# Waits of TensorE placed so that nearly every matmul has one, in a fused attention and two-layer feed-forward kernel

## Chip, cores and metric

The kernel runs on one core of a Trainium2 chip. The metric is the device time of one execution in microseconds (us), lower is better. TensorE does the matmuls and has its weight loads shown as an engine of their own (PE and PEld in the profile); VectorE is DVE, ScalarE is ACT, GpSimd is POOL, SyncE is SP.

## The reference

```python
# q, k, v: (4, 8, 576, 64)
scores = where(block_i >= block_j, 0.125 * q @ k.T, -1e9)      # blocks of 64 rows and columns
attn = exp(scores - max(scores)); attn /= sum(attn) + 1e-9
x = (attn @ v).transpose(0, 2, 1, 3).reshape(2304, 512)
h = x @ moe_w_in                                               # (512, 2048)
x = where(h >= 1, h, where(h <= -1, 0, (h + 1) ** 2 / 4)) @ moe_w_out
h = x @ moe2_w_in
out = (h * cos(h)) @ moe2_w_out
```

## The kernel before

Each operand of a matmul is split in a high and a low fp32r part, and every product is made from two or three matmuls of such parts (high by high, high by low, low by high). ACT makes the high parts, DVE or POOL the low ones.

**Attention.** A head's 576 rows are taken in two items: rows 0 to 255 (an early item, n = 0 to 31, score tiles 0 and 1) and rows 256 to 575 (a late item, n = 32 to 63, score tiles 2, 3 and 4). An item goes through `score` (queries by keys, in PSUM), row maximum (DVE), exponential with row sum (ACT, L616), reciprocal (DVE), scaling (POOL, L513), `turn` (TensorE transposes, L1019), the split of the transposed probabilities (ACT `pt_hi`, DVE `pt_lo`, L817), `weigh` (probabilities by values, L1036), and the addition of the two halves into the feed-forward's input (DVE, which then counts up `heads_read`). A late item has three transpose groups, `turn(n, 0)`, `turn(n, 1)` and `turn(n, 2)`; the third writes the PSUM tile `turned` that the first wrote. The low part of the queries is made by DVE (`q_lo_made`, L789), that of the keys by POOL (`k_lo_made`, L506).

**Feed-forward.** Tokens go in tiles of 256, t = 0 to 8 in the first layer, t = 9 to 17 in the second. The hidden dimension is taken in eight pairs of 128-blocks; a tile is 32 units on TensorE, four for a pair: two that make a hidden pair (`make_hidden`, L1090, 12 matmuls in each), and two that use one (`use_hidden`; first layer L1115, 12 matmuls in each; second layer L1107, six of 512 columns in each). Making runs two pairs ahead of using (LAG). The second layer's tiles 9 to 16 are one hardware loop.

**Order.** Every engine executes its instructions in the order in which its code is written. The steps of an item have slots in a table (AT), one table for all engines; the first nine items run alone, the others beside the tiles 0 to 6: `slots_beside` spreads the slots over half units, and TensorE calls `beside_half` in the middle (before matmul 6) and at the end of a unit. For a late item, `score` of tiles 2 and 3 is at slot 0, tile 4 at slot 7, `turn(n, 2)` at slot 19, which is slot 0 of the next item and comes before that item's scores.

## Time and profile before

| what | value |
|---|---|
| median of 3 runs | 1044.55 us (1042.11 to 1044.83) |
| the profiled execution | 1051.79 us |
| its span, first to last instruction | 1049.6 us |
| mean granted TensorE clock | 0.981 of full speed |
| instructions | 19879 |
| PE busy | 1001.9 us (95%), 7360 matmuls |
| PEld busy | 943.1 us (90%), 7360 weight loads |
| DVE, ACT, POOL busy | 657.0, 590.8, 426.5 us |

The three timed runs are taken without the profiler, the profiled execution is a further one. A matmul's row begins when its operand is read and ends by a model; rows of neighbouring matmuls overlap, so the distance between their starts is the time that one takes of the engine. A semaphore instruction's row is listed by its line and is not counted as busy.

### The profile page before, as it was taken

What the parts mean: (1) busy time and instruction counts of PE and PEld (TensorE: products, weight loads), DVE (VectorE), ACT (ScalarE), POOL (GpSimd) and SP (SyncE); (2) the same over time, 40 slices, a digit from 0 to 9 for tenths busy, and PEclk for the clock granted to TensorE, in tenths of its full rate; (3) what the DMA queues carried; (4) which work ended last, traced back from release to release, by engine and by line L of the source; (5) the groups of instructions that cost most, each with busy time, mean ns of one, the idle gap of its engine ahead of it and who ended that gap; (6) DMA issues with size and microseconds to landing.
All of it is one profiled execution on the core that took longest, in us unless ns stands there. A gap on an engine that the chain in (4) does not pass through costs nothing.

```text
span 1049.6 us, 19879 instructions
## 1 busy us (share of the span) xinstructions
PE 1001.9 (95%) x7360; PEld 943.1 (90%) x7360; DVE 657.0 (63%) x1422; ACT 590.8 (56%) x1232; POOL 426.5 (41%) x446
## 2 busy tenths in 40 slices
PE   4688999999999999999999999999999999999997
PEld 3578999999999999999999998999999999999995
DVE  5567777766766767666732378656565555656553
ACT  5567776766666666666633356544444444445442
POOL 3559765555555554655522221222222222222211
PEclk9579999999999999999999999999999999999999
DMA  4335321221211212121200144010110101001000
GB/s 133 104 118 157 98 90 65 72 70 49 92 49 53 89 49 72 70 72 65 69 31 22 41 161 162 1 40 0 40 40 0 40 0 40 21 19 40 0 21 21
DMA packets 30886, 62.28 MB, mean 59 GB/s; under 512 B 3680, under 2 KB 11872, under 8 KB 30816
## 3 DMA queue, kind: packets, MB, share of 16 engines
q1 hardware_dynamic: 29664, 57.16, 17.1%
q10 hardware_dynamic: 1152, 4.19, 1.1%
q8 instruction: 43, 0.70, 0.3%
q14 instruction: 27, 0.22, 0.1%
HBM read 51.90 MB, written 9.44 MB: 58 GB/s over the span
## 4 chain that ended last, share of the span: by engine, by line
PE 79%; DVE 9%; ACT 5%; issue 3%; POOL 1%; DMA 1%; ACTq 0%; POOLq 0%; DVEq 0%
PE hidden L1090 33%; PE acc L1107 18%; PE acc L1115 12%; PE heads_out L1036 4%; PE scores L1001 4%; PE turned L1019 3%; PE scores L1002 3%; DVE neg_max L800 1%; PE heads_out L1019 1%; DVE x_lo L879 1%; PE hidden L1073 1%; DVE wout_lo L865 1%; DVE work L885 1%; ACT probs L616 1%; DVE pt_lo L817 1%
## 5 line engine op out<-in xcount | busy, mean ns | idle before, releaser
L543 POOL TENSOR_TENSOR g_lo<-work,g_hi 128x512 fp32r<-128x512 f32 x144 | 187.9, 1305 | 450.7 <-ACT g_hi L713 450.7
L1090 PE MATMUL hidden<-x_hi,win_hi 128*128 128x256 f32 x1136 | 323.5, 285 | 2.8 <-DVE work L912 1.2
L1090 PE MATMUL hidden<-x_hi,win_lo 128*128 128x256 f32 x1136 | 317.9, 280 | 0.0
L1090 PE MATMUL hidden<-x_lo,win_hi 128*128 128x256 f32 x1136 | 317.9, 280 | 0.0
L1090 PEld LDWEIGHTS hidden<-x_hi,win_hi 128*128 128x128 f32 x1136 | 214.3, 189 | 7.6 <-issue 2.0
L1090 PEld LDWEIGHTS hidden<-x_lo,win_hi 128*128 128x128 f32 x1136 | 214.2, 189 | 3.3
L1090 PEld LDWEIGHTS hidden<-x_hi,win_lo 128*128 128x128 f32 x1136 | 216.4, 190 | 0.0
L1115 PE MATMUL acc<-g_hi,wout_hi 128*128 128x256 f32 x576 | 167.4, 291 | 0.3 <-ACT y_stage L696 0.3
L1115 PE MATMUL acc<-g_lo,wout_hi 128*128 128x256 f32 x576 | 160.6, 279 | 0.0
L1115 PE MATMUL acc<-g_hi,wout_lo 128*128 128x256 f32 x576 | 160.5, 279 | 0.0
L513 POOL TENSOR_SCALAR probs<-probs,row_inv 64x576 f32<-64x576 f32 (+2 forms) x160 | 107.4, 675 | 121.6 <-DVE row_inv L812 120.8
L723 ACT ACTIVATE work<-work 128x512 f32<-128x512 f32 x72 | 45.5, 632 | 140.3 <-DVE work L902 140.3
L616 ACT ACTIVATE probs<-scores,neg_max 64x576 f32<-64x576 f32 (+2 forms) x160 | 90.5, 567 | 58.6 <-DVE neg_max L800 56.5
L1107 PE MATMUL acc<-wout_hi,g_hi 128*128 128x512 f32 x288 | 113.7, 395 | 1.6 <-POOL g_lo L543 1.6
L1107 PE MATMUL acc<-wout_hi,g_lo 128*128 128x512 f32 x288 | 113.4, 394 | 0.0
L1107 PE MATMUL acc<-wout_lo,g_hi 128*128 128x512 f32 x288 | 112.6, 391 | 0.0
L1115 PEld LDWEIGHTS acc<-g_hi,wout_hi 128*128 128x128 f32 x576 | 108.9, 189 | 1.2 <-issue 0.4
L1115 PEld LDWEIGHTS acc<-g_lo,wout_hi 128*128 128x128 f32 x576 | 109.2, 190 | 0.6
L912 DVE TENSOR_TENSOR work<-hidden,work 128x512 f32<-128x512 f32 x72 | 49.8, 692 | 94.9 <-ACT work L725 94.9
L1115 PEld LDWEIGHTS acc<-g_hi,wout_lo 128*128 128x128 f32 x576 | 108.9, 189 | 0.0
L713 ACT ACTIVATE g_hi<-work 128x512 fp32r<-128x512 f32 x144 | 89.8, 624 | 14.7 <-DVE work L890 12.3
L800 DVE TENSOR_REDUCE neg_max<-scores 64x1 f32<-64x576 f32 (+2 forms) x160 | 86.8, 543 | 17.7 <-PE scores L1002 13.1
(91 smaller groups left out, 1830.1 us busy)
## 6 DMA issues: line engine op xcount, KB each, us to landing
qk_raw<-qk_late SPq DMA_DIRECT2D x32, 448.0 KB, 3.2
qk_raw<-qk_early SPq DMA_DIRECT2D x32, 256.0 KB, 2.6
v_raw<-v_late SPq DMA_DIRECT2D x32, 160.0 KB, 3.3
x_raw<-x_scratch SPq DMA_DIRECT2D x9, 512.0 KB, 3.5
out<-y_stage SPq DMA_DIRECT2D x36, 128.0 KB, 2.4
x_raw<-w_in SPq DMA_DIRECT2D x8, 512.0 KB, 3.6
y_stage<-w_out SPq DMA_DIRECT2D x8, 512.0 KB, 3.5
x_scratch<-y_stage ACTq DMA_DIRECT2D x8, 512.0 KB, 2.7
```

The costliest lines, as they stand in the source:

```text
L513: nc.gpsimd.tensor_scalar(tile, tile, row_inv[0:rows_of(i), col:col + 1], 1.0, ALU.mult, ALU.mult).then_inc(probs_made, 1)
L543: nc.gpsimd.tensor_tensor(g_lo[:, m % G_RING, :], work[:, m % 2, :], g_hi[:, m % G_RING, :], ALU.subtract).then_inc(g_lo_made, 1)
L616: nc.scalar.activation(tile, scores_tile(n, i), ACT.Exp, bias=neg_max[0:rows_of(i), col:col + 1], accum_out=row_sum[0:rows_of(i), col:col ...
L713: nc.scalar.activation(g_hi[:, m % G_RING, :], work[:, m % 2, :], ACT.Copy).then_inc(g_hi_made, 1)
L723: nc.scalar.activation(work[:, m % 2, :], work[:, m % 2, :], ACT.Abs).then_inc(angle_abs, 1)
L800: nc.vector.tensor_reduce(out=neg_max[0:rows_of(i), col:col + 1], in_=scores_tile(n, i), axis=AX_XY if i == 4 else AX_X, op=ALU.max, negat ...
L912: nc.vector.tensor_tensor(work[:, m % 2, :], hidden[:, m % 2, :], work[:, m % 2, :], ALU.mult).then_inc(hidden_read, 1)
L1001: nc.tensor.matmul(into, q_tile, k_hi_of(n)[:, first:end], start=True, stop=False)
L1019: last = nc.tensor.transpose(turned_of(n, e)[:, at:at + q], probs_chunk(n, i, j), ident[0:q, 0:q])
L1090: last = nc.tensor.matmul(into, w[:, p, c, half * P:(half + 1) * P], x[:, c, :], start=(i == 0), stop=(i == len(products) - 1))
L1107: last = nc.tensor.matmul(acc[:, a, :], g[:, slot, at:at + P], w[:, p, half, :], start=(p == 0 and half == 0 and i == 0), stop=(end and i ...
L1115: last = nc.tensor.matmul(into, w[:, p, half, d * P:(d + 1) * P], g[:, slot, half * TOK:(half + 1) * TOK], start=(p == 0 and half == 0 and ...
```

## The change

The waits of TensorE are placed anew; the matmuls, their order, and all other engines' code stay as they are.

- `score`: the keys' wait comes first and only ahead of an item's first tile; the queries' wait goes one matmul ahead for items from 9 on, and is left out for late items after the first, where the `pt_lo` wait of the item before (ahead of its `turn(n, 2)`) comes later in DVE's order than the queries' low part. The exponential's wait for the banks is left out where DVE's order implies it; the third tile keeps its own.
- `turn`: it waits for the scaled probabilities alone. Its second wait is left out for the first group, and goes one matmul ahead for the second (`heads_read`) and the third (`pt_lo`).
- `weigh`: the wait for `heads_read` is left out; that for the values goes one matmul ahead for items 9 to 31 and is left out for late ones.
- `make_hidden`: the wait for the activation of the pair two before (`hidden_read`) goes two matmuls ahead of the first, into the unit before. `use_hidden` of pair 0: the wait for `g_lo` goes two matmuls ahead, and the one for the accumulator (`acc_read`) stays.
- Second layer's weights: the waits at the start of the loop's body become one ahead of the loop and two single ones within it.

`steps_ahead` holds the attention's waits; it is called ahead of the matmul before a half unit's attention steps.

```diff
--- before.py
+++ after.py
@@ -111,6 +111,20 @@
 def user_before(n):
     return n - 2 if n < ALONE else n - 1
+def banks_seen(n):
+    before = n - 2 if n < ALONE else n - 1
+    last = "inv_c" if late(before) else "inv_b"
+    return n < 2 or slot_of(last, before) - sum(slots_of(m) for m in range(before, n)) <= slot_of("q_lo", n)
+def queries_seen(n):
+    return n > HEADS and slot_of("q_lo", n) + slots_of(n - 1) < slot_of("pt_lo", n - 1) and (
+        slot_of("turn_c", n - 1) <= slots_of(n - 1))
 def near(n, k):
@@ -982,15 +996,17 @@
         def _(pe):
             def score(n, i):
                 e = i - tiles_of(n)[0]
-                pe.wait_ge(q_lo_made, n + 1)
-                pe.wait_ge(k_lo_made, n + 1)
-                if late(n):
-                    pe.wait_ge(exp_made, first_tile(n) + (2 if i == 4 else 0))
-                elif n > ALONE:
-                    pe.wait_ge(exp_made, first_tile(n - 1) + e + 1)
-                elif n > 1:
-                    pe.wait_ge(exp_made, first_tile(n - 1 if n < ALONE else n))
+                if e == 0:
+                    pe.wait_ge(k_lo_made, n + 1)
+                    if kind(n) == 0:
+                        pe.wait_ge(q_lo_made, n + 1)
+                    if not banks_seen(n):
+                        pe.wait_ge(exp_made, first_tile(n))
+                elif e == 2:
+                    pe.wait_ge(exp_made, first_tile(n) + 2)
                 q_tile = q_of(n)[:, P * e:P * (e + 1)]
                 bank = bank_of(n, i)
                 if i == 4:
@@ -1005,26 +1021,37 @@
             def turn(n, e):
                 tiles = (tiles_of(n)[e],) if late(n) else tiles_of(n)
                 pe.wait_ge(probs_made, first_tile(n) + e + len(tiles))
-                if e == 1:
-                    pe.wait_ge(heads_read, n)
-                elif e == 2:
-                    pe.wait_ge(pt_lo_made, first_turn(n) + 1)
-                elif user_before(n) >= 0:
-                    pe.wait_ge(pt_lo_made, first_turn(user_before(n) + 1))
                 at = 0
-                for i, j in ([(0, 0), (1, 0), (1, 1)] if not late(n) else [(tiles[0], j) for j in range(tiles[0] + 1)]):
+                chunks = [(0, 0), (1, 0), (1, 1)] if not late(n) else [(tiles[0], j) for j in range(tiles[0] + 1)]
+                for i, j in chunks:
                     q = rows_of(i)
                     last = nc.tensor.transpose(turned_of(n, e)[:, at:at + q], probs_chunk(n, i, j), ident[0:q, 0:q])
                     at += q
                 last.then_inc(turned_made, 1)
+            def steps_ahead(n, k):
+                for m, j in near(n, k):
+                    if kind(m) != 0 and j == slot_of("score", m) and not queries_seen(m):
+                        pe.wait_ge(q_lo_made, m + 1)
+                    if kind(m) == 1 and j == slot_of("weigh", m):
+                        pe.wait_ge(v_lo_made, m + 1)
+                    if late(m) and j == slot_of("turn_b", m):
+                        pe.wait_ge(heads_read, m)
+                    if late(m) and j == slot_of("turn_c", m):
+                        pe.wait_ge(pt_lo_made, first_turn(m) + 1)
             def weigh(n):
                 pe.wait_ge(pt_lo_made, first_turn(n) + (3 if late(n) else 1))
-                pe.wait_ge(v_lo_made, n + 1)
-                if user_before(n) >= 0:
-                    pe.wait_ge(heads_read, user_before(n) + 1)
+                if kind(n) == 0:
+                    pe.wait_ge(v_lo_made, n + 1)
                 if late(n):
                     width = LATE
                     parts = [(j, LATE * j, max(P * j - EARLY, 0)) for j in range(5)]
@@ -1062,6 +1089,11 @@
                     for n, k in beside[half]:
                         attention(n, k)
+            def ahead_of_half(beside, half):
+                if beside:
+                    for n, k in beside[half]:
+                        steps_ahead(n, k)
             def begin_hidden(c):
                 pe.wait_ge(x_lo_made, c + 1)
@@ -1076,15 +1108,31 @@
                     if c == KC - 1:
                         last.then_inc(hidden_made, 1)
-            def make_hidden(t, m, half, beside=None, u=0):
+            def hidden_ahead(t, m):
+                pe.wait_ge(hidden_read, PAIRS * t + m + 1)
+            def use_ahead(t, p, first):
+                if p == 0:
+                    pe.wait_ge(g_lo_made, PAIRS * t + p + 1 + 2)
+                elif first:
+                    pe.wait_ge(wout_lo_made, p + 1)
+            def make_hidden(t, m, half, beside=None, u=0, ahead=None):
                 p = m % PAIRS
-                if half == 0:
-                    pe.wait_ge(hidden_read, PAIRS * t + m + 1)
                 into = hidden[:, m % H_BANKS, half * TOK:(half + 1) * TOK]
                 products = [(w, x, c) for c in range(KC) for w, x in ((win_hi, x_hi), (win_hi, x_lo), (win_lo, x_hi))]
                 for i, (w, x, c) in enumerate(products):
+                    if i == len(products) // 2 - 1:
+                        ahead_of_half(beside, 2 * u)
                     if i == len(products) // 2:
                         beside_half(beside, 2 * u)
+                    if i == len(products) - 2 and ahead is not None:
+                        ahead()
+                    if i == len(products) - 1:
+                        ahead_of_half(beside, 2 * u + 1)
                     if p == 0 and half == 0 and i in (0, len(products) // 2):
                         pe.wait_ge(x_lo_made, x_pieces_by(t + m // PAIRS) - (0 if i else 1))
                     last = nc.tensor.matmul(into, w[:, p, c, half * P:(half + 1) * P], x[:, c, :],
@@ -1092,17 +1140,19 @@
                 if half == 1:
                     last.then_inc(hidden_made, 1)
-            def use_hidden(t, p, half, second, beside=None, u=0):
-                if half == 0:
+            def use_hidden(t, p, half, second, beside=None, u=0, ahead=None):
+                if half == 0 and p == 0:
+                    pe.wait_ge(acc_read, t + 1)
+                elif half == 0:
                     pe.wait_ge(g_lo_made, PAIRS * t + p + 1 + 2)
-                    if p == 0:
-                        pe.wait_ge(acc_read, t + 1)
                 slot = p % G_RING
                 parts = ((wout_hi, g_hi), (wout_hi, g_lo), (wout_lo, g_hi))
                 end = p == PAIRS - 1 and half == 1
                 if second:
                     for a in range(TOK // P):
                         for i, (w, g) in enumerate(parts):
+                            if a == 1 and i == 1 and ahead is not None:
+                                ahead()
                             at = half * TOK + a * P
                             last = nc.tensor.matmul(acc[:, a, :], g[:, slot, at:at + P], w[:, p, half, :],
                                                     start=(p == 0 and half == 0 and i == 0), stop=(end and i == 2))
@@ -1111,6 +1161,12 @@
                         if d == KC // 2:
                             beside_half(beside, 2 * u)
                         for i, (w, g) in enumerate(parts):
+                            if d == KC // 2 - 1 and i == 2:
+                                ahead_of_half(beside, 2 * u)
+                            if d == KC - 1 and i == 1 and ahead is not None:
+                                ahead()
+                            if d == KC - 1 and i == 2:
+                                ahead_of_half(beside, 2 * u + 1)
                             into = acc[:, d // 2, (d % 2) * TOK:(d % 2 + 1) * TOK]
                             last = nc.tensor.matmul(into, w[:, p, half, d * P:(d + 1) * P],
                                                     g[:, slot, half * TOK:(half + 1) * TOK],
@@ -1121,30 +1177,39 @@
             def tile(t, beside=None, second=False, to_second=False, next_tile=True):
                 heads = beside is not None
+                first = heads and t == 0
+                def ahead_of(u):
+                    s = u // 4
+                    if u == UNITS:
+                        return (lambda: hidden_ahead(t + 1, LAG)) if next_tile else None
+                    if u == made_at(s, heads) - 1 and (s + LAG < PAIRS or next_tile):
+                        return lambda: hidden_ahead(t, s + LAG)
+                    if u == (made_at(s, heads) + 1 if made_at(s, heads) == 4 * s + 1 else 4 * s) and (first or s == 0):
+                        return lambda: use_ahead(t, s, first)
+                    return None
                 for u in range(UNITS):
                     s, half = u // 4, u % 2
                     m = s + LAG
-                    if second and (u % 4 == 0):
-                        for h in range(2):
-                            if s == 0:
-                                pe.wait_ge(half_lo_made[0][h], PAIRS - 1)
-                                pe.wait_ge(half_lo_made[1][h], PAIRS - 2)
-                            if s == PAIRS - LAG - 1:
-                                pe.wait_ge(half_lo_made[0][h], PAIRS)
-                            if s == PAIRS - 2:
-                                pe.wait_ge(half_lo_made[1][h], PAIRS)
+                    if second and u == 4 * (PAIRS - LAG - 1):
+                        pe.wait_ge(half_lo_made[1][1], PAIRS - 1)
+                    if second and u == 4 * (PAIRS - LAG) + 1:
+                        pe.wait_ge(half_lo_made[1][1], PAIRS)
                     if u in (made_at(s, heads) - 1, made_at(s, heads)):
                         if m < PAIRS or next_tile:
                             if to_second and m >= PAIRS and half == 0:
-                                for h in range(2):
-                                    pe.wait_ge(half_lo_made[0][h], m - PAIRS + 1)
-                            if heads and t == 0 and m < PAIRS and half == 0:
+                                pe.wait_ge(half_lo_made[0][1], m - PAIRS + 1)
+                            if first and m < PAIRS and half == 0:
                                 pe.wait_ge(win_lo_made, m + 1)
-                            make_hidden(t, m, half, beside, u)
+                            make_hidden(t, m, half, beside, u, ahead_of(u + 1))
                     else:
-                        if heads and t == 0 and half == 0:
-                            pe.wait_ge(wout_lo_made, s + 1)
-                        use_hidden(t, s, half, second, beside, u)
+                        if first and s == 0 and half == 0:
+                            pe.wait_ge(wout_lo_made, 1)
+                        use_hidden(t, s, half, second, beside, u, ahead_of(u + 1))
                     beside_half(beside, 2 * u + 1)
             pe.sem_inc(g_used, G_RING)
@@ -1153,10 +1218,12 @@
             for n in range(ALONE):
                 for k in range(slots_of(n)):
                     attention(n, k)
+            hidden_ahead(0, LAG)
             for t in range(BESIDE_TILES):
                 tile(t, slots_beside(t))
             tile(TILES - 2)
             tile(TILES - 1, to_second=True)
+            pe.wait_ge(half_lo_made[1][1], PAIRS - 2)
             with pe.Fori(TILES, 2 * TILES - 1) as t:
                 tile(t, second=True)
             tile(2 * TILES - 1, second=True, next_tile=False)
```

## Rows read from the trace of the kernel before

**Rows 1.** page, parts 1 and 4: busy time by engine; chain that ended last.
```profile
PE 1001.9 (95%) x7360; PEld 943.1 (90%) x7360; DVE 657.0 (63%) x1422; ACT 590.8 (56%) x1232; POOL 426.5 (41%) x446
...
PE 79%; DVE 9%; ACT 5%; issue 3%; POOL 1%; DMA 1%; ACTq 0%; POOLq 0%; DVEq 0%
```

**Rows 2.** windows: stretch, length, busy by engine (xinstructions), granted clock, DMA share, GB/s.
```profile
0.00:100.00 100.00, 69.27 (x408) 63.06 (x408) 63.02 (x194) 61.98 (x165) 56.23 (x76) 0.81 0.39 125
100.00:535.00 435.00, 427.16 (x3465) 413.27 (x3466) 306.59 (x840) 288.27 (x685) 252.03 (x281) 1.00 0.21 71
535.00:640.00 105.00, 105.00 (x927) 105.00 (x926) 48.87 (x71) 44.69 (x73) 24.26 (x18) 1.00 0.23 79
640.00:1050.00 410.00, 400.47 (x2564) 361.80 (x2562) 238.56 (x319) 195.84 (x310) 94.00 (x72) 1.00 0.09 26
```

**Rows 3.** by line, own wait instructions of TensorE: ns min/median/max, first, last us.
```profile
L985 PEldq EVENT_SEMAPHORE  x1: 51/51/51, 5.0 to 5.0; - x1
...
L989 PEldq EVENT_SEMAPHORE  x96: 51/51/1277, 186.2 to 526.7; - x96
...
L1013 PEldq EVENT_SEMAPHORE  x32: 51/51/51, 197.5 to 531.0; - x32
...
L1135 PEldq EVENT_SEMAPHORE  x8: 51/51/51, 674.5 to 987.7; - x8
```

**Rows 4.** timeline (start us, us, what): late third score tile, first and last.
```profile
191.77 0.20 ACT L616 ACTIVATION_READ_ACCUMULATOR probs<-scores,neg_max 128x1 f32 x1
...
192.09 0.19 PEld L1001 LDWEIGHTS scores<-k_hi,q_parts 128*128 128x128 f32 x1 [0.69 <-issue]
...
505.54 0.19 ACT L616 ACTIVATION_READ_ACCUMULATOR probs<-scores,neg_max 128x1 f32 x1
...
505.85 0.19 PEld L1001 LDWEIGHTS scores<-k_hi,q_parts 128*128 128x128 f32 x1
```

**Rows 5.** timeline, third score tile, exponential early.
```profile
234.46 0.19 ACT L616 ACTIVATION_READ_ACCUMULATOR probs<-scores,neg_max 128x1 f32 x1
...
235.25 0.28 PE L1090 MATMUL hidden<-x_hi,win_lo 128*128 128x256 f32 x1
235.26 0.19 PEld L1001 LDWEIGHTS scores<-k_hi,q_parts 128*128 128x128 f32 x1
```

**Rows 6.** timeline, late third transpose group, first and last.
```profile
251.10 0.56 DVE L817 TENSOR_TENSOR pt_lo<-turned,pt_hi 128x384 fp32r<-128x384 f32 x1
...
251.77 0.26 PEld L1019 LDWEIGHTS turned<-ident,probs 64*128 64x128 f32 x3 [0.58 <-POOL probs L513]
...
478.73 0.56 DVE L817 TENSOR_TENSOR pt_lo<-turned,pt_hi 128x384 fp32r<-128x384 f32 x1 [0.98 <-ACT pt_hi L625]
...
479.40 0.20 PEld L1019 LDWEIGHTS turned<-ident,probs 64*128 64x128 f32 x2 [0.93 <-issue]
```

**Rows 7.** timeline, third transpose group, nothing late.
```profile
208.61 0.28 PE L1115 MATMUL acc<-g_hi,wout_lo 128*128 128x256 f32 x1
...
208.82 0.39 PEld L1019 LDWEIGHTS turned<-ident,probs 64*128 64x128 f32 x5
```

**Rows 8.** timeline, first score tile that waits for the keys.
```profile
251.65 1.40 POOL L506 TENSOR_TENSOR k_lo<-qk_raw,k_hi 128x576 fp32r<-128x576 f32 x1
...
253.12 0.19 PEld L1001 LDWEIGHTS scores<-k_hi,q_parts 128*128 128x128 f32 x1 [0.96 <-issue]
```

**Rows 9.** timeline, score tile that waits for the queries.
```profile
73.30 0.46 DVE L789 SCALAR_TENSOR_TENSOR q_parts<-qk_raw,q_parts 64x256 fp32r<-64x256 f32 x1
...
73.81 0.19 PEld L1001 LDWEIGHTS scores<-k_hi,q_parts 128*128 128x128 f32 x1 [0.40 <-DVE q_parts L789]
```

**Rows 10.** timeline, hidden product that waits for the activation.
```profile
655.47 0.19 PEld L1090 LDWEIGHTS hidden<-x_hi,win_hi 128*128 128x128 f32 x1 [1.64 <-DVE work L912]
```

**Rows 11.** timeline, second layer: first of 24 hidden products, first of next group.
```profile
700.33 0.28 PE L1090 MATMUL hidden<-x_hi,win_hi 128*128 128x256 f32 x1
...
703.15 0.40 PE L1107 MATMUL acc<-wout_hi,g_hi 128*128 128x512 f32 x1
```

## The prediction

> **What bounds the kernel now.** I read the page first: PE is busy for 95% of the span, and 79% of the chain that ended last is PE's own work [rows 1]. The windows say where that holds. From 100 us on the clock is granted in full, at 2.4 GHz, and PE is busy for 427.2 of 435 us, 105 of 105, and 400.5 of 410; only the first 100 us, with 69.3 us busy and 0.81 of the clock, are a chain of dependent steps of all engines [rows 2]. So after 100 us a stall of TensorE costs what it lasts and a stall taken away gives it back, unless a later wait for another engine takes it up. ACT, DVE and POOL have room there (DVE 306.6 of 435 us). The third view is the waits: the wait instructions that stand by themselves have 19 lines in the kernel, L985 to L1135, and 425 rows, nearly all of 51 ns [rows 3]. The question is how many of these lie on the path.
>
> **Most of them are hidden.** The third score tile of item 36 has such an instruction in front of it (L989), and its weight load begins 0.01 us after the matmul before it did (235.26 after 235.25), which is the pace of a stream without any [rows 5]. I went through every score tile, transpose group and weighing in this way: whenever what it waits for was made early, the wait instruction costs nothing. It is hidden by the matmuls that wait in the queue, and it costs something only when its semaphore is what is late. The price is therefore per late semaphore, not per wait.
>
> **What a late semaphore costs in either place.** A wait that goes with the weight load: DVE ends the queries' low part at 73.76, the load begins at 73.81, 0.05 later [rows 9]. A wait with an instruction of its own: ACT ends the row sum at 191.97 and 505.73, the load begins at 192.09 and 505.85, 0.12 later [rows 4]; for `pt_lo` 251.66 to 251.77 and 479.29 to 479.40, 0.11 [rows 6]. Where the late one is the second semaphore of such an instruction it is 0.07 (253.05 to 253.12) [rows 8]. So a late wait gains 0.06 or 0.07 us, or 0.02, when it comes onto the matmul.
> The Trainium skill (Perfetto Trace Analysis, Sequencer-only Instruction) puts the semaphore wait ahead of the row that the profiler reports. The L1013 rows agree, all 51 ns although their groups stood still; the L989 rows do not, the longest has 1277 ns [rows 3]. It changes no term.
>
> **What is gained.**
> - Third score tile (wait for the exponential, now on its matmul): 19 of the 32 are late, first at 192.09, last at 505.85 [rows 4]; in the others the exponential ended about 0.6 us before [rows 5]. All 19 stood still for longer than the 0.065 that is gained, so 19 x 0.065 = 1.2 us. Bounds: nothing, if the exponential is itself held up by something that doesn't move; 1.3.
> - First score tile (wait for the keys' low part, now on its matmul): 11 are late, with 0.02 each [rows 8]: 0.2 us.
> - The accumulator's wait (`acc_read`) of tile 2: one late place, 0.06 us.
> - All waits left out (`heads_read`, the first group's `pt_lo`, the values, the second tile's keys) were early everywhere, by 0.3 us or more; they are hidden behind queued matmuls as in [rows 5] and give nothing. Nor do those in the second layer's loop, where the weights have long been split.
> Sum: 1.5 us.
>
> **What is lost.** A wait that goes ahead onto an earlier matmul holds that matmul back too, where its semaphore is late.
> - `pt_lo` ahead of the third transpose group: 10 of 32 are late, first at 251.77, last at 479.40 [rows 6]. Now the matmul before the group has to wait: its load begins 0.05 after `pt_lo`, its own start is one spacing (0.11) behind, and the group's first load comes 0.21 after that start, as where nothing is late (208.61 to 208.82) [rows 7]. That is 0.37 after `pt_lo` against 0.11 now: 0.26 lost. What is queued behind it is the group, then the next item's first score tile, which in four of the ten waits longer than that for the keys from POOL (item 38's stands idle for 0.96 us [rows 8]) and takes the loss up whole; in two more it takes up 0.06. So 4 x 0.26 + 2 x 0.20 = 1.4 us. Bounds: nothing, if the wait doesn't bite; 2.6, if nothing is taken up. I take the middle since the keys' chain (ACT, POOL) doesn't pass through this group.
> - The queries' low part one matmul ahead, items 9 to 31: three are late (73.81 [rows 9], 92.84 and 130.71), one spacing each: 3 x 0.11 = 0.3 us.
> - In the first nine items two waits remain, and the keys' is now the first named, so the queries' gets the instruction of its own: four late places, 0.065 each: 0.3 us.
> - `hidden_read` two matmuls ahead: by count, it is late once after the start, at 655.47, where the load stood idle for 1.64 us [rows 10]. The two matmuls of 512 columns before it, some 0.23 each (twice a spacing of 0.1175, below), used to run in that time: 0.46 us. Elsewhere it has 0.8 us to spare or more.
> - `g_lo` of pair 0, `heads_read` and the values' wait, moved ahead: early by 0.7 us or more, nothing; loop entry: within 0.1 either way.
> Sum: 2.5 us.
>
> **Sum.** 2.5 - 1.5 = +1.0 us on the profiled execution's 1051.8, so 1052.8. That execution is 7.2 us above the median, and I carry the difference over: 1044.55 + 1.0 = 1045.6 us. With every term at its better bound it is 1043.0, with every one at its worse 1048.3 (no gain, 2.6 + 0.3 + 0.3 + 0.5 lost).
>
> **Rivals.**
> 1. *The losses are not taken up and the gains don't last* (slower). The place is the third transpose group and the first score tile behind it: if POOL's keys come later as the group does, all ten cost 0.26, and if the exponential follows TensorE's own pace, the third score tile's stall is the same as before. Then +3.7: 1048.3. It decides from +3.1 on, so it needs nearly all of both. For it: the 10 places are there [rows 6]. Against: DVE and ACT have 30% room [rows 2]. Chance 0.19.
> 2. *The moved waits don't bite, the late ones gain* (-1.5, 1043.0): if TensorE takes the moved wait at the group after all, or the stall is given back. Against it: no row gives a reason. Chance 0.10; within 0.3%.
> 3. *The sequencer is the bound, and every wait instruction costs its 51 ns.* 425 x 0.051 = 21.7 us at most, 1023; if a third are on the path, 1037. Against it: [rows 5], and 105 us without a gap [rows 2]. The Trainium skill (TensorE: Matmul & The Clock Gate, "② Decode and dispatch") names about 62 ns of the sequencer for a matmul where hardware decoding is off. By that rule an extra instruction would show in the pace; rows 5 show it doesn't. Chance 0.07.
> 4. *The pace of the stream changes.* Two paces occur at the same granted clock: 927 matmuls in 105 us, 0.1133 each, from 535 to 640 [rows 2], and 24 from 700.33 to 703.15, 0.1175 each [rows 11], nearly all through the second layer. In the first layer the pace falls from one to the other after stalls, and which one follows depends on how a stall ends. The change shifts the last long stall (655.47) by two matmuls. If the second layer's 1,700 matmuls of this kind then run at the other pace, 1,700 x 0.0042 = 7.1 us are gained: 1038.5. Nothing says which way it falls, and it has held its pace through all group changes from 661 us on. Chance 0.14. The same in the first layer is worth 1 us either way.
>
> **How the numbers follow.** My forecast has 0.50. Within 0.3% (about 3.1 us, what a measurement of this kernel can tell from no change) also lies rival 2: 0.60. Faster: rivals 3 and 4, 0.21. Slower: rival 1, 0.19. The range reaches from rival 4 with 1 us to spare, 1037.5, to just past rival 1, 1048.8; rival 3 and what lies beyond either end are left out, some 0.15. The likeliest case alone: 1043.0 to 1048.3.
>
> **What would show it.** Right: nearly no wait instructions of TensorE's own; PE as busy as before; the third score tile's load 0.05 us behind the exponential; the last matmul before a late third transpose group 0.05 us behind `pt_lo`, and the group 0.37 behind; before 655 us the stall two L1107 matmuls earlier. Wrong: late semaphores that still take 0.12, third groups 0.11 behind `pt_lo`, or a second layer with 24 products in 2.72 us. The forecast fails above all if TensorE's stream has a cost of waits in it that shows in no start time, or if the paces change.

## The result, and the profile after

The changed kernel takes 1046.94 us (median of 13 executions, 1045.09 to 1047.96), the kernel before on the same chip 1044.55 (13, 1042.11 to 1046.28): ratio 1.0024, 95% interval 1.0016 to 1.0033. It is slower by 2.4 us. I had forecast +1.0 us and no change beyond 0.3%. The bound of 0.3% holds, but the interval lies above 1, so the loss is real, and more than half of it is something that no rival of mine had.

The page of the changed kernel, parts 1 and 4, and its windows, with the columns of [rows 1, 2]:

```profile
PE 995.6 (95%) x7360; PEld 937.5 (90%) x7360; DVE 656.7 (63%) x1422; ACT 590.4 (57%) x1232; POOL 425.8 (41%) x446
...
PE 80%; DVE 8%; ACT 6%; issue 3%; POOL 1%; DMA 1%; ACTq 0%; POOLq 0%; DVEq 0%
```
```profile
0.00:100.00 100.00, 69.80 (x427) 63.47 (x428) 64.12 (x198) 62.80 (x169) 58.45 (x78) 0.90 0.40 131
100.00:535.00 435.00, 426.73 (x3445) 412.18 (x3443) 305.04 (x835) 287.12 (x683) 249.67 (x279) 1.00 0.22 69
535.00:640.00 105.00, 104.84 (x923) 104.64 (x922) 49.54 (x72) 44.72 (x73) 24.23 (x18) 1.00 0.23 77
640.00:1050.00 410.00, 394.24 (x2571) 357.21 (x2570) 238.03 (x319) 195.73 (x310) 93.43 (x72) 1.00 0.10 27
```

From 100 to 535 us TensorE starts 20 matmuls fewer than before and from 535 to 640 us four fewer, although 388 instructions have gone (19,491 against 19,879; of TensorE's own wait instructions the trace has 32 records, and 428 before). From 640 us on it has the same work done in 394.2 us in place of 400.5. That last part is not the change's: the kernel before, profiled once more, has it too (first experiment). For that reason everything below is read against that second profile of the kernel before, which took 1043.9 us.

The places of the prediction, in the timeline of the changed kernel (start, duration, what). The third score tile, first and last late one ([rows 4] answer to them; L630 was L616, L1017 was L1001):

```profile
191.78 0.20 ACT L630 ACTIVATION_READ_ACCUMULATOR probs<-scores,neg_max 128x1 f32 x1
...
192.04 0.19 PEld L1017 LDWEIGHTS scores<-k_hi,q_parts 128*128 128x128 f32 x1 [0.62 <-ACT probs L630]
...
506.43 0.19 ACT L630 ACTIVATION_READ_ACCUMULATOR probs<-scores,neg_max 128x1 f32 x1
...
506.67 0.19 PEld L1017 LDWEIGHTS scores<-k_hi,q_parts 128*128 128x128 f32 x1
```

The row sum ends at 191.98 and 506.62, the load begins 0.06 and 0.05 later, where it was 0.12. A late third transpose group ([rows 6, 7]; L831 was L817, L1031 was L1019):

```profile
250.94 0.56 DVE L831 TENSOR_TENSOR pt_lo<-turned,pt_hi 128x384 fp32r<-128x384 f32 x1
...
251.55 0.19 PEld L1171 LDWEIGHTS acc<-g_hi,wout_lo 128*128 128x128 f32 x1 [0.62 <-DVE pt_lo L831]
...
251.87 0.38 PEld L1031 LDWEIGHTS turned<-ident,probs 64*128 64x128 f32 x5
```

`pt_lo` ends at 251.50. The matmul ahead of the group (L1171) starts 0.05 behind it and the group 0.37 behind it; it was 0.11. And the hidden product that waits for the activation ([rows 10]; L926 was L912):

```profile
654.86 0.69 DVE L926 TENSOR_TENSOR work<-hidden,work 128x512 f32<-128x512 f32 x1 [1.45 <-ACT work L739]
...
655.61 0.19 PEld L1157 LDWEIGHTS acc<-wout_hi,g_lo 128*128 128x128 f32 x1 [1.97 <-DVE work L926]
...
656.18 0.28 PE L1138 MATMUL hidden<-x_hi,win_hi 128*128 128x256 f32 x1
```

The load that stands still belongs to the second-last matmul of the group ahead, and the hidden product itself starts 0.63 us after the activation's end at 655.55; in [rows 10] its load began right behind.

So each place does what was forecast. The rest is in a place that I had not looked at: item 32, the first late one. Its queries and keys come in one transfer of 448 KB. First the changed kernel, then the second profile of the kernel before: ACT's first split of them, POOL's subtraction, and the first score tile's load.

```profile
184.41 0.47 ACT L616 ACTIVATE q_parts<-qk_raw 128x320 fp32r<-128x320 f32 x1 [1.87 <-DMA qk_raw<-qk_late]
...
185.53 1.40 POOL L520 TENSOR_TENSOR k_lo<-qk_raw,k_hi 128x576 fp32r<-128x576 f32 x1 [5.16 <-ACT k_hi L609]
...
186.99 0.19 PEld L1017 LDWEIGHTS scores<-k_hi,q_parts 128*128 128x128 f32 x1 [1.34 <-POOL k_lo L520]
```
```profile
183.94 0.47 ACT L602 ACTIVATE q_parts<-qk_raw 128x320 fp32r<-128x320 f32 x1 [0.27 <-DMA qk_raw<-qk_late]
...
185.06 1.43 POOL L506 TENSOR_TENSOR k_lo<-qk_raw,k_hi 128x576 fp32r<-128x576 f32 x1 [3.57 <-ACT k_hi L595]
...
186.57 0.19 PEld L1001 LDWEIGHTS scores<-k_hi,q_parts 128*128 128x128 f32 x1 [0.34 <-issue]
```

The brackets matter: ACT stood idle for 1.87 us for the transfer in the one and for 0.27 in the other, and TensorE's load for 1.34 us against 0.34. The DMA view of a short window inside that transfer in the changed kernel, and of one around 177 us in the kernel before, ahead of the transfer, the only time near it at which the same queue shows there (queue, kind: packets, MB, share of 16 engines). The last line of each block is from a wider window, which holds the issue of the transfer:

```profile
q1 hardware_dynamic: 83, 0.24, 48.3%
q8 instruction: 1, 0.02, 4.6%
...
qk_raw<-qk_late SPq DMA_DIRECT2D x1, 448.0 KB, 5.0
```
```profile
q8 instruction: 1, 0.02, 5.0%
...
qk_raw<-qk_late SPq DMA_DIRECT2D x1, 448.0 KB, 3.4
```

q8 carries instructions: one packet of 16 KB every 16 us or so up to 672 us, then none for 330 us while the second layer's hardware loop repeats its body; 42 in all in the changed kernel and 43 before. Outside the loop its packets keep step with TensorE (they come about 255 of its records apart on the mean), from which I take it that they fetch TensorE's instructions. In the changed kernel one starts at 181.46 us, inside the transfer, which then takes 5.0 us from issue to landing and not 3.4.

### The profile page after: what moved, and what is told of

It reads as the page before. It is cut to its first block, busy times and chain, and to the rows that moved or that the text cites. A ratio compares the mean times of both kernels' runs of the same rounds, so it can differ in the third digit from the quotient of the medians.

```text
span 1043.4 us, 19491 instructions
## 1 busy us (share of the span) xinstructions
PE 995.6 (95%) x7360; PEld 937.5 (90%) x7360; DVE 656.7 (63%) x1422; ACT 590.4 (57%) x1232; POOL 425.8 (41%) x446
## 4 chain that ended last, share of the span: by engine, by line
PE 80%; DVE 8%; ACT 6%; issue 3%; POOL 1%; DMA 1%; ACTq 0%; POOLq 0%; DVEq 0%
PE hidden L1138 33%; PE acc L1157 18%; PE acc L1171 14%; PE heads_out L1063 5%; PE scores L1017 3%; PE turned L1031 3%; PE scores L1018 3%; DVE neg_max L814 1%; DVE wout_lo L879 1%; PE heads_out L1031 1%; DVE x_lo L893 1%; ACT probs L630 1%; PE hidden L1105 1%; DVE pt_lo L831 1%; DVE work L899 1%
## 5 line engine op out<-in xcount | busy, mean ns | idle before, releaser
L1138 PEld LDWEIGHTS hidden<-x_hi,win_lo 128*128 128x128 f32 x1136 | 213.6, 188 | 3.1 <-DVE q_parts L803 1.5
L1171 PE MATMUL acc<-g_hi,wout_hi 128*128 128x256 f32 x576 | 167.6, 291 | 0.2 <-ACT y_stage L710 0.2
L1171 PE MATMUL acc<-g_hi,wout_lo 128*128 128x256 f32 x576 | 161.6, 281 | 2.5 <-DVE pt_lo L831 2.5
L1171 PE MATMUL acc<-g_lo,wout_hi 128*128 128x256 f32 x576 | 160.7, 279 | 0.0
L630 ACT ACTIVATE probs<-scores,neg_max 64x576 f32<-64x576 f32 (+2 forms) x160 | 90.4, 567 | 59.7 <-DVE neg_max L814 57.6
L1171 PEld LDWEIGHTS acc<-g_hi,wout_lo 128*128 128x128 f32 x576 | 108.9, 189 | 4.2 <-DVE pt_lo L831 4.2
L1171 PEld LDWEIGHTS acc<-g_hi,wout_hi 128*128 128x128 f32 x576 | 109.1, 189 | 1.1 <-ACT y_stage L710 0.4
L1171 PEld LDWEIGHTS acc<-g_lo,wout_hi 128*128 128x128 f32 x576 | 109.3, 190 | 0.6
L926 DVE TENSOR_TENSOR work<-hidden,work 128x512 f32<-128x512 f32 x72 | 49.8, 692 | 94.7 <-ACT work L739 94.7
```

Of the source, the lines that this page charges most:

```text
L630: nc.scalar.activation(tile, scores_tile(n, i), ACT.Exp, bias=neg_max[0:rows_of(i), col:col + 1], accum_out=row_sum[0:rows_of(i), col:col ...
L926: nc.vector.tensor_tensor(work[:, m % 2, :], hidden[:, m % 2, :], work[:, m % 2, :], ALU.mult).then_inc(hidden_read, 1)
L1138: last = nc.tensor.matmul(into, w[:, p, c, half * P:(half + 1) * P], x[:, c, :], start=(i == 0), stop=(i == len(products) - 1))
L1171: last = nc.tensor.matmul(into, w[:, p, half, d * P:(d + 1) * P], g[:, slot, half * TOK:(half + 1) * TOK], start=(p == 0 and half == 0 and ...
```

## The experiments

All 7360 matmuls stand in every trace in the same order, so one can subtract: the start of the same matmul in two traces is the lag of one against the other, and where the lag steps, time was lost. The table gives how much the lag against the second profile of the kernel before grew in each stretch (us; the stretches are cut at the starts of matmuls 1100, 1132, 3900 and 4900, at 182.7, 186.8, 537.7 and 655.9 us), and the ratio of the timed runs.

| kernel | to 182.7 | item 32 | items 32 to 63 | to 655.9 | rest | ratio (95%) |
|---|---|---|---|---|---|---|
| before, first profile | +0.54 | -0.14 | +0.11 | +0.63 | +6.77 | |
| changed | -1.13 | +1.56 | +0.92 | +0.36 | +0.01 | 1.0024 (1.0016 to 1.0033) |
| turn_c_back | +0.86 | +1.24 | -1.00 | -0.57 | +0.02 | 1.0001 (0.9986 to 1.0016) |
| hidden_back | +0.52 | +1.28 | +0.40 | -0.08 | +0.10 | 1.0013 (1.0004 to 1.0022) |
| score_only | -0.26 | -0.09 | -1.32 | -0.11 | 0.00 | 0.9983 (0.9974 to 0.9992) |
| after_shift | +2.10 | -0.18 | +0.54 | +0.37 | +0.01 | 1.0027 (1.0016 to 1.0037) |
| before_shift | +11.07 | -0.16 | +0.74 | +0.15 | 0.00 | 1.0113 (1.0098 to 1.0127) |
| latest_first | -0.59 | -0.12 | -0.69 | -0.11 | +0.02 | 1.0002 (0.9982 to 1.0021) |
| turn_c_ahead_alone | +0.24 | -0.20 | +1.59 | -0.09 | +0.03 | 1.0011 (0.9994 to 1.0028) |
| early_part | -0.12 | +1.47 | -0.08 | +0.89 | +0.02 | 1.0002 (0.9987 to 1.0017) |
| late_part | -0.99 | -0.16 | +0.88 | -0.11 | +0.02 | 1.0003 (0.9979 to 1.0027) |
| turn_c_two_ahead | +0.34 | -0.14 | +2.92 | +0.07 | +6.77 | 1.0011 (0.9985 to 1.0036) |
| scores_and_stream | -0.34 | -0.13 | -0.84 | -0.07 | +0.02 | 0.9983 (0.9968 to 0.9997) |

The first column varies by 2.0 us for the same code up to that matmul (changed, turn_c_back and early_part), so it says little. It goes in part with the clock that the first 100 us are granted: the two kernels with 0.90 have -1.1 and -1.0, the first profile of the kernel before with 0.81 has +0.5. Two profiles of the kernel before agree to 0.14 us in the next two, which can be trusted to some 0.2. The ratios are not those of the medians, long executions weigh in them, and the intervals of several are wide because some executions ran 6 to 8 us longer than the rest (the last column, see **before_again**); the table's other columns are free of that.

**before_again.** The kernel before, unchanged, profiled once more.

> The kernel before, profiled once more. Its first profiled execution had matmuls of 256 columns at about 117.8 ns all through the second layer, the changed kernel's at about 114.5 ns, which is 7 us over 656 to 1043 us. Theory A (the pace varies from execution to execution and has nothing to do with the change): this execution is near 1043 to 1046 us and shows 114.5 ns, since the timed runs of the kernel before have a median 7 us below its profiled one. Rival (the change sets the pace, my fourth case): again about 117.8 ns and about 1051 us. Also looked at: how long the transfer of the late part of queries and keys of item 32 takes (3.23 us in the first profile of before, 4.95 us after), which cost the changed kernel 1.5 us there; theory A wants it to vary here too.

1043.9 us. The same window of the second layer in the first profile of the kernel before, in its second, and in the changed kernel:

```profile
660.00:1030.00 370.00, 370.00 (x2381) 335.98 (x2380) 216.94 (x292) 178.59 (x281) 86.85 (x67) 1.00 0.08 21
```
```profile
660.00:1030.00 370.00, 369.99 (x2421) 336.45 (x2420) 219.32 (x294) 181.56 (x286) 87.60 (x68) 1.00 0.08 21
```
```profile
660.00:1030.00 370.00, 369.99 (x2421) 336.41 (x2421) 220.12 (x296) 181.02 (x286) 87.97 (x68) 1.00 0.08 21
```

In the same 370 us 2381 matmuls run in the first and 2421 in the other two; 40 more by 0.16 us (370 by 2381) are 6.2 us. The pace belongs to the execution: of 112 timed runs of the kernel before, eight took 1050 us or more. Whether the change makes such executions rarer is not settled: in the other kernels with the old waits in the stream ten of 63 were long, in the five with the changed stream (changed, turn_c_back, hidden_back, early_part, after_shift) none of 55, and in **scores_and_stream**, which has the stream of **hidden_back**, one of twelve. Item 32's transfer took 3.4 us here and 3.2 in the first profile, so the 5 us of the changed kernel were not a matter of chance, as theory A wanted it.

**turn_c_back.** One part undone:

```diff
             def turn(n, e):
                 pe.wait_ge(probs_made, first_tile(n) + e + len(tiles))
+                if e == 2:
+                    pe.wait_ge(pt_lo_made, first_turn(n) + 1)
...
             def steps_ahead(n, k):
-                    if late(m) and j == slot_of("turn_c", m):
-                        pe.wait_ge(pt_lo_made, first_turn(m) + 1)
```

> The changed kernel with one thing undone: the wait for the low part of the first transposes stands again at the third transpose group of a late item (behind the wait for the probabilities) and no longer one matmul ahead. My theory (a late wait costs what is in front of it, about 0.26 us for each of some 10 late groups, of which some is taken up behind): the groups' gap of about 0.69 us falls back to 0.32 us with the matmul before at 0.11, and the kernel is about 1.4 us faster than the changed one, ratio to before 1.0010. Rival 1 (none of the losses is taken up): 2.6 us faster, ratio 1.0000. Rival 2 (moved waits do not bite at all): as the changed kernel, ratio 1.0024.

1044.23 us, 1.0001. In items 32 to 63 it is 1.92 us faster than the changed kernel (-1.00 against +0.92), by the trace. The timed ratio went from 1.0024 to 1.0001, with 0.0015 to either side, and cannot tell 1.9 us from the first rival's 2.6; the trace can, four of the ten groups' losses are taken up behind them. The group's load is 0.11 behind `pt_lo` again:

```profile
252.48 0.56 DVE L831 TENSOR_TENSOR pt_lo<-turned,pt_hi 128x384 fp32r<-128x384 f32 x1
...
253.15 0.38 PEld L1033 LDWEIGHTS turned<-ident,probs 64*128 64x128 f32 x5 [0.58 <-POOL probs L527]
```

**hidden_back.** The other part undone:

```diff
             def make_hidden(t, m, half, beside=None, u=0, ahead=None):
+                if half == 0:
+                    pe.wait_ge(hidden_read, PAIRS * t + m + 1)
...
                 def ahead_of(u):
-                    if u == UNITS:
-                        return (lambda: hidden_ahead(t + 1, LAG)) if next_tile else None
-                    if u == made_at(s, heads) - 1 and (s + LAG < PAIRS or next_tile):
-                        return lambda: hidden_ahead(t, s + LAG)
...
```

> The changed kernel with the wait for the hidden products read back at the first matmul that overwrites them, on that matmul, and no longer two matmuls ahead. My theory: the one stall of 1.9 us near 655 us ends on the matmul and not two before it, 0.3 to 0.46 us gained, nothing else moves: ratio to before 1.0019 to 1.0021, which timing can hardly tell from the changed kernel's 1.0024, but the trace can. Rival (these waits, one in each of 16 groups of the second layer and in each first-layer group, cost something each even when long satisfied): 2 us or more faster, ratio about 1.000. The pace of the second layer says whether the place of this wait sets it: by my theory 114.5 ns as before it.

1045.67 us, 1.0013. At the one stall (matmuls 4880 to 4900) the lag grows by 0.36 us in the changed kernel, by 0.46 in **early_part**, which has the same wait, and by 0.02 here: 0.34 to 0.44, as forecast or a little less. The other waits of this kind cost nothing: the second layer is the same within 0.1. Item 32 loses 1.28 us here too, and 1.24 in **turn_c_back**. In all three kernels the transfer takes 3.3 to 3.6 us from its first packet to its last, with a packet of q8 inside; in the two profiles of the kernel before 2.0 and 2.1, with none.

**score_only.** One part of the change put into the kernel before:

```diff
-                pe.wait_ge(q_lo_made, n + 1)
-                pe.wait_ge(k_lo_made, n + 1)
-                if late(n):
-                    pe.wait_ge(exp_made, first_tile(n) + (2 if i == 4 else 0))
-                elif n > ALONE:
+                if i == 4:
+                    pe.wait_ge(exp_made, first_tile(n) + 2)
+                else:
+                    pe.wait_ge(q_lo_made, n + 1)
+                    pe.wait_ge(k_lo_made, n + 1)
+                    if late(n):
+                        pe.wait_ge(exp_made, first_tile(n))
+                    elif n > ALONE:
...
```

> The kernel before with one part of the change: the third score tile of a late item waits for its exponential alone and on its own matmul; queries and keys, which the item's first tile has waited for, are not named there again. All else as before. My theory: 19 late third tiles cost 0.14 in place of 0.23 us, net 0.06 us each: 1.2 us faster than before, ratio 0.9988. Rival 1 (what a tile gains, the next wait takes back): ratio 1.0000. Rival 2 (each instruction left out is worth its own 0.1 us of the sequencer, late or not): 28 or more by 0.1, 3 us or more, ratio 0.997.

1042.42 us, 0.9983, faster than the kernel before with the whole interval. Nineteen third tiles start 0.09 sooner and the matmul behind them gives 0.03 back. That is 19 x 0.065 = 1.24 us. Of the -1.32 in the table 0.34 fall at one other place, 328 us, so that some 1.0 of the 1.24 lasts, and 0.24 is lost again elsewhere (0.14 of it at the transpose group at 402 us). At 328 us it was POOL's L519 that took 0.88 us in place of 1.36 in **before_again**; why is open.

**after_shift** and **before_shift.** Instructions that only fill TensorE's stream, in the changed kernel and in the kernel before (there with 18 in place of 9):

```diff
                         score(m, tiles_of(m)[0])
                         score(m, tiles_of(m)[1])
+                        for _ in range(9 if m < 9 else 0):
+                            pe.sem_inc(unread, 1)
```

> The changed kernel with 81 more instructions in TensorE's stream, nine behind the scores of each of the first nine items, where TensorE waits anyway: each adds one to a semaphore that nobody reads. The first runs gave a new theory (F): TensorE's instructions come in by fetches of 16 KB (DMA queue q8, one each 15 us or so). In the changed kernel and its two variants a fetch falls inside the 448 KB transfer of item 32's queries and keys, which then takes 3.3 to 3.6 us in place of 2.0, and TensorE loses 1.2 to 1.5 us there; in the kernel before, with more instructions ahead of that place, the fetch comes 5 us before the transfer. By F the 81 instructions bring the fetch to about 176.9 us, the transfer takes 2.0 us again, and this kernel is 1.2 to 1.5 us faster than the changed one, ratio 1.0010 to 1.0013. Rival (the loss at item 32 comes from the moved waits there, the keys' or the queries'): the fetch moves, but item 32 still loses 1.2 us or more against the kernel before, ratio 1.0024 as the changed kernel.

> The kernel before with 162 more instructions of the same sort, 18 behind the scores of each of the first nine items. By theory F they bring the fetch that came at 193.2 us to about 182.5 us, into item 32's transfer: the transfer takes 3.3 us or more in place of 2.0, and the kernel is 1.2 to 1.5 us slower than before, ratio 1.0012 to 1.0015, if the added instructions cost nothing of their own in the first 70 us. Rival (waits, not fetches, made that loss): ratio 1.0000 and the stall at item 32 as before.

The 81 instructions cost more than they were to bring: 1046.6 us and 1.0027, since they are not all hidden in the first nine items (+2.10 us to 182.7, 3.2 more than in the changed kernel and 1.2 more than in **turn_c_back**, which has the same code there). But item 32 is clear: its lag grows by -0.18 us and not by +1.56, and the transfer takes 3.2 us. The fetch starts at 179.2 us, 4.4 us ahead of the first packet of the transfer:

```profile
q8 instruction: 1, 0.02, 4.3%
...
qk_raw<-qk_late SPq DMA_DIRECT2D x1, 448.0 KB, 3.2
```

The moved waits of item 32 are all still there, so the rival falls. The second kernel missed: the 162 instructions cost 11 us, everything behind came later, and the fetch fell at 194.3 us on the last packets of a transfer that had begun at 192.6. That transfer took no longer. It says only that a fetch at the tail of a transfer does no harm.

**early_part** and **late_part.** The change cut in two by items. **early_part** is the changed kernel with every wait of items 32 to 63 as before, **late_part** the kernel before with only these changed. The core of each:

```diff
 early_part, against the changed kernel
                 e = i - tiles_of(n)[0]
-                if e == 0:
+                if late(n):
+                    pe.wait_ge(q_lo_made, n + 1)
+                    pe.wait_ge(k_lo_made, n + 1)
+                    pe.wait_ge(exp_made, first_tile(n) + (2 if i == 4 else 0))
+                elif e == 0:
...
 late_part, against the kernel before
+                if late(n):
+                    if e == 0:
+                        pe.wait_ge(k_lo_made, n + 1)
+                        if not banks_seen(n):
+                            pe.wait_ge(exp_made, first_tile(n))
+                    elif e == 2:
+                        pe.wait_ge(exp_made, first_tile(n) + 2)
+                else:
+                    pe.wait_ge(q_lo_made, n + 1)
+                    pe.wait_ge(k_lo_made, n + 1)
...
```

> The changed kernel with all waits of the late items (32 to 63: score tiles, transpose groups, weighing) as in the kernel before; the change stays in items 0 to 31 and in the stream of the hidden and output products. Up to item 32 TensorE's stream has as few instructions as the changed kernel (29 waits in instructions of their own, the kernel before 149). Theory F (a fetch of TensorE's instructions falls into item 32's transfer): 1.2 to 1.5 us lost at item 32, and 0.45 us by the stall moved two matmuls ahead at 655 us, nothing in the late items: ratio to before 1.0015 to 1.0019. Rival (the moved waits of item 32 itself make the loss there): only the 0.45 us stays, ratio 1.0004.

> The other half alone: the kernel before with the change in the waits of items 32 to 63 only. Up to item 32 the stream has the 149 waits of its own of the kernel before, so the fetch falls 5 us ahead of item 32's transfer. Theory F: nothing lost at item 32; in the late items, score tiles -1.3 us, third transpose groups +1.6 us, queries' waits and the pace of the stream (113 or 118 ns, whichever it falls into behind a stall) +0.3 to +0.9: in all +0.6 to +1.2 us against before, ratio 1.0006 to 1.0012. Rival (item 32's own waits): 1.2 to 1.5 us more, all of it at item 32, ratio 1.0018 to 1.0026.

The table is plain. **early_part** has item 32's waits as the kernel before has them, and loses 1.47 us there; **late_part** has them as the changed kernel has them, and loses nothing. What decides is how many instructions stand in front, and with them where the packet of q8 falls. All fourteen traces side with that: in the four with a packet inside the first 1.1 us of item 32's transfer (changed, turn_c_back, hidden_back, early_part) it takes 3.3 to 3.6 us from first packet to last and item 32 loses 1.24 to 1.56 us; in the other ten it takes 1.8 to 2.1 us and item 32 loses nothing. The row of ACT in **early_part**, 1.77 us idle for the transfer, and its DMA:

```profile
185.32 0.47 ACT L616 ACTIVATE q_parts<-qk_raw 128x320 fp32r<-128x320 f32 x1 [1.77 <-DMA qk_raw<-qk_late]
...
q8 instruction: 1, 0.02, 1.8%
...
qk_raw<-qk_late SPq DMA_DIRECT2D x1, 448.0 KB, 4.8
```

The late items alone lose 0.88 us, the changed kernel 0.92. **early_part** also loses 0.43 us from 640 to 647 us, where the first profile of the kernel before lost 0.6 and the changed kernel nothing; at the change of layers the lag varies by half a microsecond (**turn_c_back** has -0.57 there), which I didn't follow up. The ratios, 1.0002 and 1.0003, are below what was expected (1.0015 and 1.0006 at least); their intervals hold it. Five of the 29 executions of the kernel before that they are measured against were long ones; the medians, 1045.7 and 1044.9 against 1044.7, lie 1.0 and 0.2 us above it.

**turn_c_ahead_alone** and **turn_c_two_ahead.** The kernel before with only `pt_lo`'s wait moved, one and two matmuls ahead of the group (the lines of the second; in the first both `- 2` are `- 1`; likewise among the output products):

```diff
             def turn(n, e):
-                elif e == 2:
-                    pe.wait_ge(pt_lo_made, first_turn(n) + 1)
...
                 for i, (w, x, c) in enumerate(products):
+                    if i == len(products) // 2 - 2:
+                        ahead_of_half(beside, 2 * u)
+                    if i == len(products) - 2:
+                        ahead_of_half(beside, 2 * u + 1)
...
```

> The kernel before with one part of the change alone: the wait for the low part of the first transposes stands one matmul ahead of each third transpose group, not at it. The number of instructions stays, so the fetches stay where they were. My theory, with the size now taken from the traces of the changed kernel and of its variant with this undone (six late groups at 0.25 us, the others nearly taken up; 1.9 us between the two over all late items): 1.5 to 1.9 us slower than before, ratio 1.0014 to 1.0018. Rival (the losses of the changed kernel needed its other moves): ratio 1.0000.

> The kernel before with the wait for the low part of the first transposes two matmuls ahead of the third transpose group (one matmul ahead alone lost 1.6 us between items 32 and 63 by the trace). My theory (a late wait costs what stands between it and its user): each of the six groups that paid 0.25 us pays one matmul more, 0.11, and some groups that were just in time now are late: 2.3 to 3.0 us lost there, ratio 1.0020 to 1.0030. Rival (the cost is that the wait stands alone, not how far ahead it is): 1.6 us as with one matmul, ratio 1.0011 to 1.0015.

+1.59 and +2.92 us in the late items: the distance is what costs. In the second, item 37's group starts 0.48 us behind `pt_lo` (251.51), one spacing more than the 0.37 of one matmul ahead:

```profile
250.95 0.56 DVE L817 TENSOR_TENSOR pt_lo<-turned,pt_hi 128x384 fp32r<-128x384 f32 x1
...
251.56 0.19 PEld L1128 LDWEIGHTS acc<-g_lo,wout_hi 128*128 128x128 f32 x1 [0.74 <-DVE pt_lo L817]
...
251.99 0.38 PEld L1017 LDWEIGHTS turned<-ident,probs 64*128 64x128 f32 x5
```

The timed medians, 1045.1 and 1046.7 against 1043.9 and 1044.7 of the kernel before, go the same way, with intervals that hold no change.

**latest_first.** The kernel before with **score_only**'s edit, the keys named ahead of the queries, and at the third group

```diff
+                if e == 2:
+                    pe.wait_ge(pt_lo_made, first_turn(n) + 1)
                 pe.wait_ge(probs_made, first_tile(n) + e + len(tiles))
-                elif e == 2:
-                    pe.wait_ge(pt_lo_made, first_turn(n) + 1)
```

> The kernel before with no wait moved to another instruction; only the order in which waits are named, and what is named twice, changes: the third score tile waits for its exponential alone, a first or second score tile names the keys first, and the third transpose group names the low part of the first transposes first and the probabilities second. My theory (a late wait costs 0.05 us when it is the one on the weight load and 0.11 to 0.12 in an instruction of its own): the third tiles give 1.2 us as in the run of that part alone, some 10 late third transpose groups 0.06 each, the late keys 0.06 each in some 10 items: 2.0 to 2.4 us faster than before, ratio 0.9977 to 0.9981. Rival (only the number of instructions counts, not which wait is named first): as the third score tiles alone, whose trace gained 1.3 us, ratio 0.9987.

The median is 1.3 us below the kernel before's, the ratio, with three executions of twelve over 1048, 1.0002 (0.9982 to 1.0021); the 2.0 to 2.4 us that I expected did not come. At its places the edit works: in six of the ten late groups the load begins 0.05 us behind `pt_lo` and no longer 0.12, two are late no more, and in the other two the probabilities come as late as `pt_lo`. First this kernel, then **before_again**:

```profile
304.07 0.55 DVE L817 TENSOR_TENSOR pt_lo<-turned,pt_hi 128x384 fp32r<-128x384 f32 x1
...
304.67 0.32 PEld L1021 LDWEIGHTS turned<-ident,probs 64*128 64x128 f32 x4 [0.29 <-DVE pt_lo L817]
```
```profile
305.06 0.55 DVE L817 TENSOR_TENSOR pt_lo<-turned,pt_hi 128x384 fp32r<-128x384 f32 x1
...
305.73 0.39 PEld L1019 LDWEIGHTS turned<-ident,probs 64*128 64x128 f32 x5 [0.36 <-issue]
```

And yet the late items gain only 0.69 us, 0.63 less than **score_only**. The ten groups give 0.1 us in all, counted from three matmuls ahead of each to nine behind: the next spacing gives 0.03 back, and the score tile behind takes up more. And the stream has two spacings there, 113.3 and 118 ns, and changes between them at stalls. Summed over the spacings of 110 to 122 ns between 256-column matmuls of these items, the difference from 113.3 ns comes to 3.71 us here, 3.18 in **score_only**, 3.08 in **before_again**, 3.79 in the changed kernel. So 0.5 us of the 0.63 is the pace. Why it differs is not shown; a stall that ends 0.09 us sooner or later may be enough for the stream behind it to go on at the other spacing.

**scores_and_stream.** Two parts of the change that had not cost anything: **score_only**'s edit, and the stream's waits as in **hidden_back**.

> The kernel before with two parts of the change that the runs so far found cheap or good: the third score tile of a late item waits for its exponential alone, and the waits in the stream of hidden and output products (weights' low parts, loop entry, g_lo ahead of acc_read) as in the changed kernel, but the wait for the hidden products read on the first matmul of its group. The waits of the scores, transposes and weighings otherwise as before, so the fetch comes 4.5 us or more ahead of item 32's transfer. My sum: the scores' 1.3 to 1.4 us, the stream 0.0: ratio 0.9983 to 0.9988, as the scores alone. Also looked at: whether the 117.8 ns pace of the second layer, which adds 7 us to some executions of the kernel before (7 of its 95 timed ones so far) and of variants with its stream (10 of some 60), but to none of 55 with the changed stream, stays away here too. If the pace has nothing to do with the stream's waits, one or two of 11 executions should be near 1049 us.

1042.46 us, 0.9983, interval 0.9968 to 0.9997. It is no better than **score_only**, and one execution of twelve took 1048.1, so these stream waits don't keep the long executions away by themselves. Of the kernels run, **score_only** is the simpler of the two fastest: one function's waits, 1.8 us (0.17%) faster than the kernel before and, by the two ratios, some 4.3 faster than the changed one.

## Why the forecast was near and its reasons incomplete

- *The price of a late semaphore* (0.05 on the load, 0.11 to 0.12 in an own instruction, a hidden one nothing): right, in every place looked at. 388 instructions fewer gave no time of their own (**score_only**'s gain is at its 19 tiles, rival 3 is out).
- *Gains 1.5 us*: third score tiles 1.2; they give 1.24 at their places, and 1.0 of it lasts (**score_only**). The keys' tiles 0.02 each: in **latest_first** they start 0.05 sooner and the next matmul gives 0.03 back, in six places.
- *`pt_lo` ahead, 1.4 us*: measured 1.59 alone; 1.92 as the difference of **turn_c_back**, of which 0.37 is pace. Six groups pay 0.25 each and the other four next to nothing, as I had them.
- *`hidden_read`, 0.46*: 0.34 to 0.44.
- *Queries' waits, 0.6 us in items 0 to 31*: not to be resolved; executions of one kernel differ by more than that before 182 us.
- *Rivals 1 and 2*: both are out. The losses are taken up in four of ten groups and most of the gains last, against the first; the moved waits bite in every one of the ten groups (0.37 behind `pt_lo`, it was 0.11 or 0.12), against the second.
- *Rival 4, the pace of the second layer*: I had taken the 117.8 ns of one profile for the kernel's own. It is an execution's: the first profile of the kernel before showed it and the second did not. As a cause it is out, and the step "I carry the difference over" was right only because of that. In the late items, where I had said that the pace "is worth 1 us either way" and put nothing into the sum, it took 0.7 us from the changed kernel.
- *The step that failed* is the sentence "All waits left out ... give nothing". They give nothing where they stand, but they are instructions, and leaving 120 of them out ahead of item 32 moved the fetch of the next 16 KB into the one transfer that TensorE is waiting for. That costs 1.2 to 1.6 us. It was shown from both sides: the loss goes when instructions are put in (**after_shift**) and stays when item 32's own waits are put back (**early_part**), and item 32's waits alone don't bring it (**late_part**).

That the whole stayed within 0.3% is in part luck: what the sum had priced, the queries' waits aside, came to +0.7 to +0.9 us, and the two things that it had at nothing, the fetch and the pace, to 2.3 us.

The account by the table: item 32 +1.56, late items +0.92 (scores -1.0 to -1.2, keys -0.1, groups +1.6, pace +0.7), `hidden_read` and the accumulator's wait +0.36: +2.84 us, and +2.4 measured. The difference lies within what the first 180 us vary by.

That the fetch delays the transfer is shown; how is not. Its packet takes 0.96 us in the changed kernel, on one of 16 engines (4.6% of them in the 1.3 us of that window), and the transfer is late by 1.5. Later fetches also fell into such transfers (in the changed kernel items 34, 40, 43, 49, 52, 58 and 61, 2.5 to 3.0 us from first to last packet), where the keys have time to spare and the lag shows no step that the groups don't explain.

## What to carry to other kernels

Price a wait by whether its semaphore is late and by what stands between it and its user; count late ones, not waits. A wait moved ahead by one matmul costs that matmul each time it is late (0.25 us here), and saves nothing where it is early. When instructions are added or left out, look at where the instruction fetches fall against the transfers that are only just in time, and profile the kernel before twice before a difference of pace is believed.

## What the runs showed of the hardware that I had not expected

- TensorE's instructions come in by packets of 16 KB on a DMA queue of their own, one for about 255 of its records on the mean and none within the second layer's loop, those near item 32 0.9 to 1.8 us long. Inside item 32's transfer of 448 KB such a packet stretched it from 2.0 us to 3.3 to 3.6 from first to last packet (four kernels). Over all late items of the fourteen traces it matters where the packet falls: in 37 transfers it began between 0.2 us ahead of their first packet and 1.1 us behind it, and they took 2.4 to 4.5 us; in 41 it began 1.3 us behind it or later, and 32 of them took 1.6 to 2.3 us, as those without one do (1.97 in the median, 361 of 362 at most 2.42).
- At the full granted clock the same stream of 256-column matmuls runs at 113.3 or at 118 ns. In the attention's part which one follows a stall is the same in both profiles of the kernel before; in the second layer it differed between executions (379.6 or 386.3 us from the start of matmul 4900 to that of the last) and explains the executions of 1050 us, as far as two profiles of that sort tell.
- An instruction that adds one to a semaphore is not free where TensorE has idle time (it is busy for 68.3 of the first 100 us in **before_again**): in the first nine items 162 of them cost 11 us, 0.07 each.
